# Attention sums copied unscaled, their rows scaled by VectorE and their columns by GpSimd, with the steps of the token mix left where they are

## What is computed

```python
# attention: 2 batches, 8 heads, 768 tokens, 64 dims; keys kept: the first 8, or 0 <= rel < 96
scores = q @ k.T / sqrt(D) + bias(distance, head);  scores = where(keep, scores, -1e9)
a = exp(scores - max);  a = a / (sum(a) + 1e-9);  x = a @ v       # x: [2, 768, 512] over all heads
# mixer and channel network
u = x + (x.T @ U @ V).T                                            # rank 32, over the tokens
x = u + relu(u @ w_ch1) @ w_ch2
# gated network with a spatial product
u, v = split(relu(x @ w_in));  v = w_spatial @ normalise(v) + b
out = (u * v) @ w_out
```

## Time and profile before

| what | value |
|---|---|
| median of 3 runs | 499.96 us (499.73, 499.96, 501.85) |
| profiled execution | 499.4 us, its span 497.4 us |
| busy: PE / DVE / ACT / POOL | 97% / 62% / 45% / 51% of the span |
| granted TensorE clock | 1.0 of full speed |
| attention stage on TensorE | first scores 6.5 us, last `weigh` from 95.60 us |
| PE in 40 slices, in tenths (12.4 us each) | 8889899799999999999999999999999999999997 |
| POOL in 40 slices | 6978666454335776735586456231886200950000 |

### The profile page before, as it was taken

The page is one execution under the profiler, slowest core; times in us unless marked ns, Lnnn a source line. Parts: engine busy times, 40 slices in busy tenths (PEclk is TensorE's granted clock), DMA queues, the critical chain, the costliest instruction groups (busy, mean ns, idle before and its releaser), DMA issues.

```text
span 497.4 us, 7981 instructions
## 1 busy us (share of the span) xinstructions
PE 483.4 (97%) x2756; PEld 403.8 (81%) x2756; DVE 308.4 (62%) x731; ACT 224.5 (45%) x519; POOL 251.4 (51%) x222
## 2 busy tenths in 40 slices
PE   8889899799999999999999999999999999999997
PEld 8678578587888888888888888888888888998986
DVE  6878679421259455564565646557878888888600
ACT  7889879542235543341332413315352356333122
POOL 6978666454335776735586456231886200950000
DMA  5565643232222420222130120220212000001022
GB/s 177 177 184 164 191 144 86 78 126 86 85 84 86 169 86 5 81 84 85 50 120 20 66 86 1 86 63 0 65 63 82 36 1 1 2 0 43 21 86 105
DMA packets 19113, 39.48 MB, mean 79 GB/s; under 512 B 3840, under 2 KB 7168, under 8 KB 19072
## 3 DMA queue, kind: packets, MB, share of 16 engines
q1 hardware_dynamic: 17056, 35.55, 21.7%
q10 hardware_dynamic: 2016, 3.41, 1.8%
HBM read 35.75 MB, written 3.19 MB: 78 GB/s over the span
## 4 chain that ended last, share of the span: by engine, by line
PE 68%; DVE 8%; POOL 8%; DMA 5%; ACT 4%; issue 3%; SPq 3%; DVEq 2%; POOLq 0%; ACTq 0%
PE bank L1885 15%; PE bank L1819 9%; PE bank L1743 9%; PE bank L1967 8%; PE bank L1914 8%; PE bank L1907 8%; PE bank L1610 7%; DMA inv_rows<-inv_scratch 2%; SPq L428 2%; DMA inv_scratch<-inv_T 2%; ACT prob L1265 1%; POOL sp_op L650 1%; PE bank L1668 1%; DVEq L1094 1%; POOL qk_split L544 1%
## 5 line engine op out<-in xcount | busy, mean ns | idle before, releaser
L595 POOL TENSOR_TENSOR w_slot<-stage,w_slot 128x1024 fp32r<-128x1024 f32 x30 | 73.3, 2453 | 65.7 <-ACT w_slot L1341 65.7
L1026 DVE TENSOR_TENSOR uT<-bank,uT 128x512 f32<-128x512 f32 x68 | 45.8, 690 | 25.3 <-PE bank L1914 23.2
L1265 ACT ACTIVATE prob<-prob,row_min 128x256 f32<-128x256 f32 (+1 forms) x96 | 46.2, 483 | 3.9 <-DVE row_min L822 3.4
L1885 PE MATMUL bank<-u_op,s_slot 128*128 128x512 f32 x192 | 47.6, 389 | 0.0
L1819 PE MATMUL bank<-hid,w_slot 128*128 128x512 f32 x192 | 46.9, 393 | 0.0
L1743 PE MATMUL bank<-u_split,w_slot 128*128 128x512 f32 x192 | 46.4, 391 | 0.0
L1907 PE MATMUL bank<-hid,w_slot 128*128 128x512 f32 x192 | 46.1, 389 | 0.0
L1914 PE MATMUL bank<-hid,w_slot 128*128 128x512 f32 x192 | 46.1, 389 | 0.0
L1064 DVE TENSOR_TENSOR part<-part,bank 128x512 f32<-128x512 f32 x40 | 27.5, 686 | 26.9 <-PE bank L1885 26.5
L1819 PEld LDWEIGHTS bank<-hid,w_slot 128*128 128x128 f32 x192 | 35.7, 188 | 8.2 <-issue 0.9
L1885 PEld LDWEIGHTS bank<-u_op,s_slot 128*128 128x128 f32 x192 | 36.0, 188 | 7.5
(11 more groups left out here) (154 smaller groups left out, 945.1 us busy)
## 6 DMA issues: line engine op xcount, KB each, us to landing
stage<-in_w_ch SPq DMA_DIRECT2D x30, 512.0 KB, 3.3
qk_raw<-in_qk SPq DMA_DIRECT2D x23, 256.0 KB, 3.6
v_all<-in_v SPq DMA_DIRECT2D x12, 256.0 KB, 3.5
inv_rows<-inv_scratch SPq DMA_DIRECT2D x48, 64.0 KB, 2.7
out_dram<-o_stage ACTq DMA_DIRECT2D x11, 256.0 KB, 2.0
stage<-in_w_spT SPq DMA_DIRECT2D x6, 384.0 KB, 3.2
stage<-in_w_in SPq DMA_DIRECT2D x4, 512.0 KB, 3.7
stage<-in_w_ch SPq DMA_DIRECT2D x8, 128.0 KB, 3.3
```

The source lines that it names most:

```text
L595: nc.gpsimd.tensor_tensor(dst[:, LO, :], stage[n % 2][:, 0:w], dst[:, HI, :].bitcast(F32), ALU.subtract).then_inc(w_lo, 1)
L1026: vec.tensor_tensor(y, y_bank(e)[:], y, ALU.add).then_inc(y_sum, 1)
L1265: last = sc.activation(prob[r][:, e, 0:w], prob[r][:, e, 0:w], ACT.Exp, bias=row_min[:, k:k + 1], scale=-1.0, accum_out=row_sum[:, q:q + 1])
L1885: last = mm(seven_bank[held][:], lhs, u_op[op][:, m, k, :], start=not more and k == 0 and p == 0, stop=k == 1 and p == 2, skip_group_check ...
```

## The change

In words, by engine:

- VectorE copies the sums of every quad unscaled into `uT` (`copy_o(s)`, in step `s` itself, no wait for the table), and takes the rows of `x_all` out of `x_bank`, scaled by the reciprocals with a broadcast (`take_x(s)`). It also adds 1e-9 to the row sums. It no longer copies `probT` but for quads 0 and 1.
- GpSimd scales `uT` in place once the table is there (`scale_u(g - 2)` in its step `g`, before `split_qk(g + 4)`; the last two after its loop), and counts `x_late`.
- ScalarE copies both halves of `probT` and no longer makes `take_x` and `add_eps`.
- TensorE's `turn_x` comes one step earlier, `turn_x(s - 1)` in step `s`; one more of them lies in the attention stage, and the last one, quad 23, right behind the first product of the channel network.
- SyncE's `spread_inverse(g)` waits for GpSimd's scaling of quad `g - 3`. `sum_u` waits for `x_late`.
- `GATHER` and `MIX_AT` stay at 14 and 16, 18, 20, 20.

```diff
                 sp.wait_ge(inv_out[g % 2], 16 * (g // 2 + 1))
-                if g == 3:
-                    sp.wait_ge(x_late, 1)
-                elif g > 3:
-                    sp.wait_ge(xT_sb, g - 2)
+                if g >= 3:
+                    sp.wait_ge(x_late, g - 2)
                 for e in range(2):
...
 
-            def scale_late():
-
-                pool.wait_ge(inv_in[0], 32)
-                pool.wait_ge(x_ps, 1)
-                nc.gpsimd.tensor_tensor(x_tile(0), x_tile(0), inv_rows[0][:], ALU.mult).then_inc(x_late, 1)
+            def scale_u(g):
+
+                pool.wait_ge(inv_in[g % 3], 32 * (g // 3 + 1))
+                pool.wait_ge(x_ps, g + 1)
+                nc.gpsimd.tensor_tensor(x_tile(g), x_tile(g), inv_rows[g % 3][:], ALU.mult).then_inc(x_late, 1)
 
             def round_V():
...
                         copy_k(g + 3)
+                    if g >= 2:
+                        scale_u(g - 2)
                     if 6 <= g + 4 < QUADS:
                         split_qk(g + 4)
-                    if g == 1:
-                        scale_late()
                     if g == 6:
                         round_V()
...
                         if g == MIX_AT[j] + 2:
                             split_u(j)
+                scale_u(QUADS - 2)
+                scale_u(QUADS - 1)
...
                 w = 2 * P * blocks(g // 2)
-                if g < 2:
-
-                    dve.wait_ge(turned, 2 * g + 1)
-                    vec.tensor_copy(probT[2 * g][:, 0:w], pt_bank[0][:, 0:w]).then_inc(probT_a, 1)
+                dve.wait_ge(turned, 2 * g + 1)
+                vec.tensor_copy(probT[2 * g][:, 0:w], pt_bank[0][:, 0:w]).then_inc(probT_0, 1)
                 dve.wait_ge(turned, 2 * g + 2)
-                if g >= 2:
-                    dve.wait_ge(pv_done, g - 1)
-                vec.tensor_copy(probT[(2 * g + 1) % 4][:, 0:w], pt_bank[1][:, 0:w]).then_inc(probT_d, 1)
+                vec.tensor_copy(probT[2 * g + 1][:, 0:w], pt_bank[1][:, 0:w]).then_inc(probT_1, 1)
 
             def invert(g):
                 q = slice(g % 4 * 4, g % 4 * 4 + 4)
+                if g == 0:
+                    dve.wait_ge(inv_set, 4)
+                dve.wait_ge(expd, 2 * g + 2)
+                vec.tensor_tensor(row_one[:, q], row_sum[:, q], eps[:], ALU.add).then_inc(sum_eps, 1)
                 dve.wait_ge(sum_eps, g + 1)
-                if g == 0:
-                    dve.wait_ge(inv_set, 3)
                 if g >= 3:
                     dve.wait_ge(inv_turned, g - 2)
-                if g == 3:
-                    dve.wait_ge(x_half, 1)
+                    dve.wait_ge(x_half, g - 2)
                 vec.reciprocal(row_inv[g % 3][:, :, 0].rearrange("p (e m) -> p m e", e=2),
                                row_one[:, q].rearrange("p (m e) -> p m e", e=2)).then_inc(inv_ok, 1)
 
...
 
-            def copy_o():
-
-                dve.wait_ge(pv_done, 1)
-                vec.tensor_copy(x_tile(0), x_bank(0)[:, 0:256].rearrange("p (c q) -> p c q", c=2)).then_inc(xT_sb, 1)
-
-            def take_x0():
-
-                dve.wait_ge(x_ps, 1)
-                vec.tensor_tensor(x_all[:, 0, 0:256].rearrange("p (m e d) -> p m e d", m=2, e=2),
-                                  x_bank(0)[:, 0:256].rearrange("p (m e d) -> p m e d", m=2, e=2),
-                                  row_inv[0][:, :, 0].rearrange("p (e m) -> p m e", e=2).unsqueeze(3).to_broadcast([P, 2, 2, D]),
+            def copy_o(g):
+
+                dve.wait_ge(pv_done, g + 1)
+                vec.tensor_copy(x_tile(g), x_bank(g)[:, 0:256].rearrange("p (c q) -> p c q", c=2)).then_inc(xT_sb, 1)
+
+            def take_x(g):
+
+                t, hq = divmod(g, 2)
+                dve.wait_ge(x_ps, g + 1)
+                if t == XS and hq == 0:
+                    dve.wait_ge(z_acc, 1)
+                vec.tensor_tensor(x_all[:, t % XS, hq * 256:hq * 256 + 256].rearrange("p (m e d) -> p m e d", m=2, e=2),
+                                  x_bank(g)[:, 0:256].rearrange("p (m e d) -> p m e d", m=2, e=2),
+                                  row_inv[g % 3][:, :, 0].rearrange("p (e m) -> p m e", e=2).unsqueeze(3).to_broadcast([P, 2, 2, D]),
                                   ALU.mult).then_inc(x_half, 1)
-
-            def scale_x(g):
-
-                dve.wait_ge(inv_in[g % 3], 32 * (g // 3 + 1))
-                dve.wait_ge(pv_done, g + 1)
-                vec.tensor_tensor(x_tile(g), x_bank(g)[:, 0:256].rearrange("p (c q) -> p c q", c=2),
-                                  inv_rows[g % 3][:], ALU.mult).then_inc(xT_sb, 1)
 
             def split_z(b):
...
                 dve.wait_ge(mixed, j + 1)
+                dve.wait_ge(x_late, (8, 12, 16, 24)[j // KD])
                 vec.tensor_tensor(u, mix_bank(j)[:, 0:end - first], u, ALU.add).then_inc(u_sum, 1)
...
                     vec.memset(row_inv[r][:], 0.0).then_inc(inv_set, 1)
-                for s in range(-2, QUADS + 1):
+                for s in range(-2, QUADS):
                     if s + 2 < QUADS:
                         score_bias(s + 2, 0)
                         if s < 1:
                             score_bias(s + 2, 1)
-                    if 0 <= s + 1 < QUADS:
-                        if s < 1:
-                            take_probT(s + 1)
-                        invert(s + 1)
-                        turn_inverse(s + 1)
-                    if s == QUADS - 2:
-                        take_probT(s + 1)
-                    if s == 1:
-                        copy_o()
-                    if s >= 2:
-                        scale_x(s - 1)
-                    if s == 15:
-                        split_z(0)
-                    if s == MIX_AT[0]:
-                        dve.wait_ge(x_late, 1)
                     for j in range(FIRST):
                         if s == MIX_AT[j]:
                             sum_u(j)
-                    if s >= 1:
-                        if s + 2 < QUADS:
-                            score_bias(s + 2, 1)
-                        if s + 1 < QUADS - 1:
-                            take_probT(s + 1)
-                        if s == 1:
-                            take_x0()
+                    if s in (-1, 0):
+                        take_probT(s + 1)
+                    if 0 <= s + 1 < QUADS:
+                        invert(s + 1)
+                    if s >= 0:
+                        copy_o(s)
+                    if s == GATHER + 1:
+                        split_z(0)
+                    if s >= 1 and s + 2 < QUADS:
+                        score_bias(s + 2, 1)
+                    if 0 <= s + 1 < QUADS:
+                        turn_inverse(s + 1)
+                    if s >= 0:
+                        take_x(s)
             with dve.Else():
                 dve.sem_inc(w_o, 1)
...
                 w = 2 * P * blocks(g // 2)
+                act.wait_ge(pv_done, g - 1)
                 act.wait_ge(turned, 2 * g + 1)
-                act.wait_ge(pv_done, g - 1)
-                sc.activation(probT[2 * g % 4][:, 0:w], pt_bank[0][:, 0:w], ACT.Copy).then_inc(probT_a, 1)
-
-            def add_eps(g):
-                q = slice(g % 4 * 4, g % 4 * 4 + 4)
-                act.wait_ge(expd, 2 * g + 2)
-                if g >= 4:
-                    act.wait_ge(inv_ok, g - 3)
-                sc.activation(row_one[:, q], row_sum[:, q], ACT.Copy, bias=1e-9).then_inc(sum_eps, 1)
-
-            def take_x(g):
-
-                t, hq = divmod(g, 2)
-                act.wait_ge(x_ps, g + 1)
-                if t == XS and hq == 0:
-                    act.wait_ge(z_acc, 1)
-                sc.activation(x_all[:, t % XS, hq * 256:hq * 256 + 256], x_bank(g)[:, 0:256],
-                              ACT.Copy).then_inc(x_half, 1)
+                sc.activation(probT[2 * g % 4][:, 0:w], pt_bank[0][:, 0:w], ACT.Copy).then_inc(probT_0, 1)
+                act.wait_ge(turned, 2 * g + 2)
+                sc.activation(probT[2 * g % 4 + 1][:, 0:w], pt_bank[1][:, 0:w], ACT.Copy).then_inc(probT_1, 1)
 
             def wide_take_xT(g):
                 act.wait_ge(w_xT_ps, g + 1)
...
-                            add_eps(g)
                     if s == GATHER + 1:
                         round_z(0)
                     if s >= 1:
                         take_probT(s + 1)
-                        if s >= 2:
-                            take_x(s - 1)
                     if 1 <= s and g < QUADS and s != GATHER:
                         exps(g, 1)
-                        add_eps(g)
                     if s == -1:
                         set_bias(2)
...
                         turn(s)
-                    if s >= 2:
-                        turn_x(s - 2)
+                    if s >= 1:
+                        turn_x(s - 1)
                     if s == GATHER + 1:
                         pe.wait_ge(z_copy, 1)
...
                 hidden(0)
-                turn_x(QUADS - 2)
+                turn_x(QUADS - 1)
             with pe.Else():
```

20 lines of the change are left out of this document (8 added, 12 removed).

## The result

The changed kernel takes 507.19 us (median of runs from 506.58 to 508.79) against 500.9 of the kernel before beside it: ratio 1.0131, interval 1.0092 to 1.017. It is slower, by 6.3 us between the medians, where the forecast had 501.0 and a range of 497.5 to 504.5. The profiled execution took 506.58 us with a span of 504.5, against 499.4 and 497.4: the spans differ by 7.1 us, and that is what is accounted for here.

The account below looks back on a forecast made before the run. In the attention stage, the table's way through DRAM was taken to bound single steps, TensorE the others. Terms 2.3 - 2.8 + 0.5 + 1.1 + 0.1 - 0.2 - 0.35 + 0.25 = +0.9 on 499.96: about 501.0 us, range 497.5 to 504.5.

Parts of the forecast that it names:

- GpSimd in front of quad 9: Up to `weigh(9)`: scalings and table waits fill GpSimd, so quad 9 is weighed near 45.2; +2.3 us (0.2 to 3.4).
- Quads 10 to 15: TensorE's step bounds again; waits at quads 10 to 12 and one for `take_x` go: -2.8 us.
- ScalarE +0.5: `weigh` needs both `probT` copies from ScalarE, which arrives late around steps 11 to 13: +0.5 us (0 to 0.6).
- The chain that a rival made the bound: ScalarE's exponentials and two copies, from `scores(s + 2)` to `weigh(s + 1)`; if 0.1 over, +2 us: 503; chance 0.10.
- `split_z`, +1.1: VectorE's queue behind `take_x(14)` delays `split_z`, for which `scores(18)` waits: +1.1 us (0.6 to 1.3).
- Quads 17 to 23 and the end of the stretch: GpSimd full again, its ends set by ScalarE's roundings: +0.1 us at quad 19, -0.2 at the end.
- The pair of transposes -0.35: One pair of transposes leaves the full stretch behind 96.63 us: -0.35 us.
- the weights +0.25: Behind 96.63, SyncE's queue reaches its weight load behind a table sent 0.4 us later: +0.25 us (0 to 0.5).
- Start: Quad 0's `turn_x` pair starts at 14.9 us, about 2.2 us of TensorE idle, the delay hidden by what follows.
- the table that gates GpSimd: Rival: every wait of a full GpSimd for a table goes to the end, six at 0.7 us: 504.5 us; chance 0.23.

Follow-up runs that it names:

- The run without a table: Changed kernel with each GpSimd scaling multiplying the tile by itself, without waiting for the table: 502.58 us, ratio 1.0022.
- The run with six products: Changed kernel with 6 unread identity products on TensorE in front of weighing quads 7, 8, 9 and 23: 505.06 us, ratio 1.008.
- the run with fourteen: Changed kernel with 14 unread identity products on TensorE in front of weighing quads 7, 8, 9 and 23: 510.12 us, ratio 1.0185.
- the runs for the add and for the tail: Changed kernel with 1e-9 added on ScalarE again: 505.34 us; changed kernel with `copy_v(23)` ahead of the last `split_u` pair: 504.26 us.
- the three together: Changed kernel with 1e-9 on ScalarE, GpSimd's scaling behind `split_qk`, and `copy_v(23)` ahead of the last splits of u: 500.59 us, ratio 1.0003.

## Why the prediction was wrong, by its steps

- **GpSimd in front of quad 9: forecast +2.3 (0.2 to 3.4), measured +4.06. This is the first step that failed.** The mechanism, the place (waits at `weigh(7)` to `weigh(9)`, 5.6 us for 3 to 4) and the work were right: 25.9 us for 26.4. Two sizes weren't. The waits for tables came to 3.55 us where the middle had about 2.2 and its upper end 2.8 (1.0 + 1.8). One of them, 0.63 for quad 0's table, wasn't in the sum at all, and quad 4's table let the scaling begin at 32.65, when 31.5 had been taken from the kernel before. It was sent 0.54 us later (27.31 for 26.77), and from there to its use it took 5.34 us for 4.73. And the term took the stretch's idle time as all usable, though 1.07 us of it are gaps between GpSimd's own instructions, as 1.1 of the 4.2 us were in the kernel before. 16.4 + 25.93 + 3.55 + 1.07 = 46.95. The run without a table won 2.5 us there, or some 3.3 by the estimate above, which agrees.
- **Quads 10 to 15: -2.8 and ScalarE +0.5.** From `weigh(9)` to `turn(16)` the difference shrinks by 1.50, with 1.53 us in it of a slow clock (46.95 to 51.58 is 4.63 us; the same step took 3.10 in the kernel before, 42.89 to 45.99): -3.03 without it. The gain was right; ScalarE cost nothing, TensorE has no wait for its `probT` copies. The chain that a rival made the bound isn't one.
- **`split_z`, +1.1:** +1.46 from `turn(16)` to `turn(17)`, in waits of 0.62 for `copy_o` and 0.56 for `z_stack`. Right in place, about right in size.
- **Quads 17 to 23 and the end of the stretch: +0.1 - 0.2, measured +2.22 (4.02 to 6.24). The second step that failed.** "The 1e-9 on VectorE costs a small add, inside its slack of 0.3 us a step", put at 0, is the sentence: the add is held while GpSimd works, mean 0.5 us and up to 1.85, and `copy_o` stands behind it, which now has less than one step to TensorE. The run with the 1e-9 on ScalarE takes exactly these three waits away. By place, 1.57 of the 2.22 us arise up to `weigh(22)` (96.69 for 91.10), where waits of 0.60, 0.97 and 1.12 for `copy_o` stand against 0.77 and 0.68 for others before. The tail adds 0.48 up to `weigh(23)`: `copy_v(23)` stands behind a `split_u` pair that waits 3.08 us for ScalarE, and makes a wait of 2.32, where the kernel before, with the same pair waiting 3.11, had 1.12 and 0.83. The last 0.17 is the clock. That "the waits at quads 21 to 23 stay" held for the kernel before's order, in which the sums had a step more.
- **No term at all for the clock.** It gave 1.53 us behind quad 9 and 1.40 in `hidden(0)` (4.42 for 3.02), 2.93 in the trace. The run with six products won 2.1 us back in the median, not all of it from the clock; the run with fourteen shows the clock and not its price. As the profiled execution of the kernel before happened to have no low stretch, the difference of the two spans holds the whole of it, and the one of the medians less.
- **The pair of transposes -0.35 and the weights +0.25:** the last checkpoints go from +7.64 to +7.1, -0.54. The weights didn't wait, as TensorE came later by more than SyncE's queue; the early `copy_v(23)` shows the term where TensorE comes sooner (1.35).
- **Start:** forecast at 14.9 with 2.2 us of wait; 14.73 with 1.87. Right.
- **Slips in the sums, without weight:** the way of the table, 1.65 + 1.1 + 2.7, is 5.45 us and not 5.2; `weigh(9)` "all at its longest" is 42.9 + 0.2 + 2.8 = 45.9 and not 46.3; six scalings at VectorE's price, 6 x 0.42, are 2.5 us and not 2.2; and `split_z`, 6.7 us against 5.9 less 0.5, is +1.3, nearer to the +1.46 measured than the +1.1 taken.

Sum of the measured: 4.06 - 1.50 + 1.46 + 2.22 + 1.40 - 0.54 = 7.10. Against the forecast's +0.9 that is 6.2 more: +1.8 at quad 9, +2.9 by the clock, +2.3 by the late waits, -0.5 that ScalarE didn't take, -0.3 in the rest.

Of the rivals, the table that gates GpSimd came nearest in time (504.5), but not by its own reckoning: not six small waits of 0.7 but three, one of them 2.37; two later ones (2.40 at 57.74, 1.88 at 68.37) fell where GpSimd had room. The removal of the waits on the table in steps 10 to 15, the reason for which a gain was to be had, took place in full. It was paid for three times elsewhere.

What stays open: why the table of quad 4, sent 0.54 us later, also took 0.6 us longer to land was not tried by itself; and the runs for the add and for the tail (2.0 and 2.9 us of span) differ from the kernel after in the number of low stretches of the clock too, three and one for two, so they show which waits go and not what each is worth.

## What to carry to other kernels

An engine that arrives just in time has a budget made of its work, its waits and its gaps: add all three before giving it a new job, and remember that the new wait holds everything queued behind it. A chain that gets one step shorter turns each small instruction ahead of it into a candidate for the critical path, so the smallest one moved to another engine has to be looked up by what runs beside it there. And work moved out of a full stretch only pays where the new place is shown to be empty.

## What the runs showed of the hardware

**A short add on VectorE is held by GpSimd.** 128x4 in fp32 takes 0.15 us at its shortest and up to 1.85 while GpSimd works, in both forms: two inputs in SBUF, or one and a constant. Its neighbours in the queue never were held; all 24 of each in the kernel after, by shortest, median and longest in ns:

```profile
L842 DVE TENSOR_TENSOR row_one<-row_sum,eps x24: 151/362/1848, 11.2 to 98.2; 128x4 f32<-128x4 f32 x24
L847 DVE RECIPROCAL row_inv<-row_one x24: 179/180/182, 11.3 to 98.4; 128x4 f32<-128x4 f32 x24
L860 DVE COPY uT<-bank x24: 391/394/425, 14.3 to 103.0; 128x256 f32<-128x256 f32 x24
L855 DVE STREAM_TRANSPOSE inv_T<-row_inv x24: 301/306/313, 11.6 to 98.8; 128x128 f32<-128x128 f32 x24
```

The Trainium skill, "SBUF — State Buffer", section "Who interferes with whom", has an exclusive lock on a port pair that the two engines share, held for a whole instruction. For the two-input form the trace agrees: every held add ends with an instruction of GpSimd. The add of 93.90 moreover was not let in between two instructions of GpSimd but waited for both (94.50, 95.73), and there the measurement goes beyond one instruction; those of 81.88 and 90.08 were let in behind one (83.02, 91.22), although the next started at once. What decides between the two isn't shown.

**TensorE's clock fell after it had stood still, but not each time.** It was 0.66 over 47 to 52 us behind waits of 1.61, 2.05 and 1.96 us, 0.71 over 103 to 108 behind waits of 0.97, 1.12 and 2.32, and 1.00 in both places where products filled them. Each of the two low stretches lost some 1.5 us (4.63 for 3.10, 4.42 for 3.02). Whether a given wait brings one isn't fixed. The wait of about 2 us in front of 14.7 us, which every run with the changed order has, was followed by 1.00 over 12 to 20 us in the kernel after and in the run with the early `copy_v(23)`, and by 0.79 over the same stretch in the run without a table and the three together. The kernel before, 1.00 throughout in its profiled execution, isn't free of it: of its 92 executions beside the experiments 12 had a mean clock of 1.000 and a median span of 497.5 us, 58 had 0.996 or 0.997 and 498.8, and 16 had 0.993 and 500.3. So a sum made on one profiled execution carries an uncertainty of some 1.5 us for each low stretch that it happens to have.
